# Channel attention folded into a two-MLP kernel: half of the fold moved between the first quad's products, the first tokens loaded during the gram, and up weights prepared quad by quad

## The reference

```python
# q, k, v: (1, 6016, 256); both MLPs: 256 -> 2048 -> 256
qn = q / (np.linalg.norm(q, axis=1, keepdims=True) + 1e-06)
kn = k / (np.linalg.norm(k, axis=1, keepdims=True) + 1e-06)
s = kn.transpose(0, 2, 1) @ qn / tau          # 256 x 256
a = np.exp(s - s.max(-1, keepdims=True)); a /= a.sum(-1, keepdims=True) + 1e-09
x = (v @ a).reshape(6016, 256)
x = np.square(np.maximum(x @ moe_w_in, 0.0)) @ moe_w_out
h = x @ moe2_w_in
y = np.maximum(0.01 * h, h) @ moe2_w_out
```

## Time and profile before

| | |
|---|---|
| median of 3 runs | 1052.86 us (1052.44 to 1053.63) |
| the profiled execution's own time | 1053.86 us |
| its span, first to last instruction | 1052.1 us |
| PE / DVE / ACT busy | 1026.6 / 735.7 / 673.0 us (98% / 70% / 64%) |
| mean granted TensorE clock | 0.995 |
| DMA | 69.24 MB, mean 66 GB/s |

### The profile page before, as it was taken

The page is one execution under the profiler, slowest core; times in us unless marked ns, Lnnn a source line. Parts: engine busy times, 40 slices in busy tenths (PEclk is TensorE's granted clock), DMA queues, the critical chain, the costliest instruction groups (busy, mean ns, idle before and its releaser), DMA issues.

```text
span 1052.1 us, 13051 instructions
## 1 busy us (share of the span) xinstructions
PE 1026.6 (98%) x4590; PEld 862.5 (82%) x4590; DVE 735.7 (70%) x1168; ACT 673.0 (64%) x1156; POOL 0.8 (0%) x7
## 2 busy tenths in 40 slices
PE   7978999999999999999999999999999999999998
PEld 6856788888888888888888888888888888888886
DVE  6887766766766666666656767767767767767665
ACT  6667767777777777777766555555555555555553
POOL 0000000000000000000000000000000000000000
PEclk9998999999999999999999999999999999999999
DMA  8730011203103113014436002002002001000001
GB/s 294 256 117 22 30 48 42 75 25 129 62 35 133 45 51 134 31 65 149 165 114 205 1 1 79 1 1 74 5 1 70 9 1 66 14 0 20 20 1 41
DMA packets 32400, 69.24 MB, mean 66 GB/s; under 512 B 2640, under 2 KB 16976, under 8 KB 32336
## 3 DMA queue, kind: packets, MB, share of 16 engines
q1 hardware_dynamic: 32336, 68.43, 19.2%
HBM read 44.56 MB, written 23.86 MB: 65 GB/s over the span
## 4 chain that ended last, share of the span: by engine, by line
PE 94%; DVE 2%; DMA 2%; ACT 1%; issue 1%; SPq 0%; ACTq 0%; DVEq 0%
PE bank L421 30%; PE bank L423 30%; PE bank L422 30%; PE bank L428 3%; DMA raw<-in_vT 1%; DMA qk<-in_k 1%; DVE xop_lo L846 0%; ACT win_hi L610 0%; DVE win_lo L872 0%; DVE g L990 0%; DVE wi_lo L777 0%; DVE wout_lo L877 0%; ACT wi_hi L576 0%; DVE folded L913 0%; ACT L580 0%
## 5 line engine op out<-in xcount | busy, mean ns | idle before, releaser
L672 ACT ACTIVATE g_hi<-g 128x496 fp32r<-128x496 f32 (+1 forms) x384 | 237.3, 618 | 208.5 <-DVE g L947 76.5
L937 DVE TENSOR_TENSOR g_lo<-g,g_hi 128x496 fp32r<-128x496 f32 (+1 forms) x384 | 260.1, 678 | 145.7 <-ACT g_hi L672 144.9
L421 PE MATMUL bank<-g_hi,wout_hi 128*128 128x496 f32 (+1 forms) x768 | 296.5, 386 | 0.0
L422 PE MATMUL bank<-g_lo,wout_hi 128*128 128x496 f32 (+1 forms) x768 | 296.3, 386 | 0.0
L423 PE MATMUL bank<-g_hi,wout_lo 128*128 128x496 f32 (+1 forms) x768 | 296.2, 386 | 0.0
L421 PE MATMUL bank<-xop_hi,win_hi 128*128 128x496 f32 (+1 forms) x672 | 260.8, 388 | 11.5 <-DVE g L990 9.0
L422 PE MATMUL bank<-xop_lo,win_hi 128*128 128x496 f32 (+1 forms) x672 | 259.9, 387 | 0.0
L423 PE MATMUL bank<-xop_hi,win_lo 128*128 128x496 f32 (+1 forms) x672 | 259.9, 387 | 0.0
L422 PEld LDWEIGHTS bank<-g_lo,wout_hi 128*128 128x128 f32 x768 | 144.5, 188 | 27.0
L423 PEld LDWEIGHTS bank<-g_hi,wout_lo 128*128 128x128 f32 x768 | 144.4, 188 | 27.1
L421 PEld LDWEIGHTS bank<-g_hi,wout_hi 128*128 128x128 f32 x768 | 144.5, 188 | 27.0
(11 more groups left out here) (99 smaller groups left out, 670.7 us busy)
## 6 DMA issues: line engine op xcount, KB each, us to landing
up_parts<-park_up SPq DMA_DIRECT2D x8, 896.0 KB, 4.4
qk<-in_q SPq DMA_DIRECT2D x15, 384.0 KB, 3.7
qk<-in_k SPq DMA_DIRECT2D x15, 384.0 KB, 5.1
stage_o<-in_w_out SPq DMA_DIRECT2D x16, 256.0 KB, 3.8
down_parts<-park_down SPq DMA_DIRECT2D x8, 512.0 KB, 2.9
raw<-in_vT SPq DMA_DIRECT2D x8, 496.0 KB, 5.9
x_tiles<-out_buf SPq DMA_DIRECT2D x8, 496.0 KB, 2.8
raw<-x_tiles SPq DMA_DIRECT2D x8, 496.0 KB, 4.2
```

Of the source, the lines that this page charges most:

```text
L421: pe.matmul(out, a_hi, b_hi, start=start and i == 0, stop=False, **more)
L422: pe.matmul(out, a_hi, b_lo, start=False, stop=False, **more)
L672: act.activation(g_hi[:, tile, 0:W], g[:, tile, 0:W], ACT.Copy).then_inc(g_hi_made[tile], 1)
L937: dve.tensor_tensor(g_lo[:, tile, 0:W], g[:, tile, 0:W], g_hi[:, tile, 0:W].bitcast(F32), ALU.subtract).then_inc(g_split[tile], 1)
```

## The change

- The tokens of group 0 (`raw0`, two DMAs of 512 KB) are loaded during the gram, after the tenth chunk; those of group 1 as soon as the gram is ready. Both have places of their own in SBUF; w_in1 gets four stage buffers in place of three, and its four loads wait for nothing.
- The sums of squares (L455 before) are put on PE before the last gram chunk, and `q_row` before the last gram tile. DVE copies `q_row` to SBUF (`q_bc`) and makes the scaled gram in one instruction a block in place of two. Six matmuls whose result nobody reads (`KEEP_WARM`) stand between the gram and the transposes.
- PE runs only units 0 to 3 of the fold before window 0. Units 4 to 7 stand between window 0's products, each of which waits only for the token block and the weights that it reads.
- `folded` is laid out by quad, and `up_add`, `up_high`, `up_low` work on one quad: 128 and 384 elements in place of 256 and 512+256; quad 0 before window 0, quad 1 in it, and quad n+1 in window n. Of the scaling, DVE keeps one unit and ACT takes seven. The second MLP's quads go through the same functions.
- The blocks of tokens are split in another order (`SPLIT_ORDER`), that in which window 0 reads them. Group 1's sums are made from window 1 on.

```diff
-STAGES = 3
+KEEP_WARM = 6
 CHUNK = 1024
-EARLY_CHUNKS = 2
...
-SPLIT_ORDER = (B11, B21, B22, T1, T2, T4, T3)
+SPLIT_ORDER = (B11, T1, T2, B21, T3, B22, T4)
+SUM_ORDER = (T1, T2, T3, T4)
...
-            with sp.Fori(1, QK_ROUNDS) as r:
+            def load_raw0():
+                for j in range(2):
+                    sp.dma_start(raw0[:, 2 * j:2 * j + 2, 0:width(0)], vT_b[:, :, tokens(0, j)]).then_inc(raw_loaded, 16)
...
-                for slot in range(QK_SLOTS):
-                    c = r * QK_SLOTS + slot
-                    sp.wait_ge(chunk_used, c - QK_SLOTS + 1)
-                    sp.wait_ge(chunk_squared, c - QK_SLOTS + 1)
-                    load_chunk(c, slot)
+            for c in range(QK_SLOTS, QK_CHUNKS):
+                sp.wait_ge(chunk_used, c - QK_SLOTS + 1)
+                sp.wait_ge(chunk_squared, c - QK_SLOTS + 1)
+                load_chunk(c, c % QK_SLOTS)
+                if c == 2 * QK_SLOTS - 1:
+                    load_raw0()
...
-                if n >= STAGES:
-                    sp.wait_ge(w_split, n - STAGES + 1)
...
-            sp.wait_ge(gram_ready, 1)
-            load_raw(0)
             load_down(0)
             load_down(1)
+            sp.wait_ge(gram_ready, 1)
+            load_raw(1)
             load_up(0)
...
+                if slot == QK_SLOTS - 1:
+                    pe.wait_ge(constants, 2)
+                    pe.wait_ge(chunk_added, QK_CHUNKS + 1 + QK_TILES)
+                    for i in range(2):
+                        for b in range(CB):
+                            last = pe.matmul(sums[:, i, b, :], sq_sum[:, i, 0, b * P:(b + 1) * P], ones[:, 0:2],
+                                             start=True, stop=True)
+                    last.then_inc(sums_ready, 1)
...
+            gram_tile(edge[:, 0, 1, :], edge[:, 1, 1, :], False, True).then_inc(gram_ready, 1)
+
+
+            pe.wait_ge(w_hi, 1)
+            for i in range(KEEP_WARM):
+                pe.matmul(fold[0], wi1_hi[:, 0, 0:P], wi1_hi[:, 0, 0:UNIT], start=True, stop=True)
...
+            def wait_weights(Q, split):
+                G, quad = divmod(Q, QUADS)
+                if G == 0:
+                    pe.wait_ge(up_split, 2 * quad + split)
+
...
+            def first_window():
+                W = width(0)
+                def x_ready(part):
+                    pe.wait_ge(x_split, SPLIT_ORDER.index(part) + 1)
+                wait_weights(0, 1)
+                x_ready(B11)
+                pe.wait_ge(fold_scaled[0], 1)
+                product(0, bank_a[:, 0:W], A11, B11, True).then_inc(p1_ready, 1)
+                fold_unit(4)
+                wait_weights(0, 2)
+                x_ready(T1)
+                pe.wait_ge(fold_scaled[1], 1)
+                product(0, bank_c[:, 0:W], S1, T1, True).then_inc(p5_ready, 1)
+                fold_unit(5)
+                x_ready(T2)
+                pe.wait_ge(seeded, 1)
+                product(0, bank_d[:, 0:W], S2, T2, False).then_inc(u2_ready, 1)
+                x_ready(B21)
+                product(0, bank_a[:, 0:W], A12, B21, False).then_inc(c11_ready, 1)
+                fold_unit(6)
+                x_ready(T3)
+                pe.wait_ge(u2_kept, 1)
+                product(0, bank_d[:, 0:W], S3, T3, False).then_inc(u3_ready, 1)
+                x_ready(B22)
+                pe.wait_ge(p5_kept, 1)
+                product(0, bank_c[:, 0:W], S4, B22, False).then_inc(p35_ready, 1)
+                fold_unit(7)
+                x_ready(T4)
+                pe.wait_ge(c22_made, 1)
+                product(0, bank_d[:, 0:W], A22, T4, False).then_inc(c21_ready, 1)
+
+
             def window(Q):
                 G, quad = divmod(Q, QUADS)
                 W = width(G)
...
+            for u in range(UNITS // 2):
+                fold_unit(u)
...
+            x_high(0, 0)
+            weights_hi(0)
+            weights_hi(1)
+            act.wait_ge(sums_ready, 1)
+            act.activation(norm[:, :, :], sums[:, :, :, 0], ACT.Sqrt).then_inc(rooted, 1)
+            act.activation(warm[:, 1:2], ones[:, 0:1], ACT.Exp)
+            x_high(0, 1)
+            weights_hi(2)
+            weights_hi(3)
...
+                act.wait_ge(e_inv_ready, 1)
+                x_high(0, 2)
+                x_high(0, 3)
+                fold_scale(0, 0)
+                up_high(0)
+                fold_scale(1, 0)
+                up_sums_high(0)
+                act.wait_ge(p1_ready, 1)
+                act.wait_ge(fold_scaled[0], 2)
+                act.activation(bank_d[:, 0:W], bank_a[:, 0:W], ACT.Copy).then_inc(seeded, 1)
+                fold_scale(1, 1)
+                x_high(0, 4)
+                x_high(0, 5)
+                act.wait_ge(p5_ready, 1)
+                act.activation(p5[:, 0:W], bank_c[:, 0:W], ACT.Copy).then_inc(p5_kept, 1)
+                act.wait_ge(u2_ready, 1)
+                act.activation(u2[:, 0:W], bank_d[:, 0:W], ACT.Copy).then_inc(u2_kept, 1)
+                x_high(0, 6)
+                up_high(1)
+                act.wait_ge(c11_ready, 1)
+                square(0, C11, bank_a, c11_relu)
+                fold_scale(2, 0)
+                fold_scale(2, 1)
+                g_high(0, C11)
+                down_high(0)
+                up_sums_high(1)
+                g_high(0, C22)
+                fold_scale(3, 0)
+                act.wait_ge(c21_ready, 1)
...
+            def up_add(n):
+                a11, a12, a22, a21 = (up_blocks(n)[:, i, :] for i in range(4))
+                s1, s2, s3, s4 = (wsum[:, n % 2, i, :] for i in range(4))
+                if n < QUADS:
+                    dve.wait_ge(fold_scaled[0], n // 2 + 1)
+                    dve.wait_ge(fold_scaled[1], n // 2 + 1)
+                else:
+                    dve.wait_ge(up_loaded, 32 * (n - QUADS + 1))
+                dve.tensor_tensor(s1, a21, a22, ALU.add).then_inc(up_sums, 1)
+                dve.tensor_tensor(s3, a11, a21, ALU.subtract).then_inc(up_sums, 1)
+                dve.wait_ge(up_sums, 4 * n + 1)
+                dve.tensor_tensor(s2, s1, a11, ALU.subtract).then_inc(up_sums, 1)
+                dve.wait_ge(up_sums, 4 * n + 3)
...
+            weights_lo(1)
+            dve.wait_ge(q_row_ready, 1)
+            dve.tensor_copy(q_bc[:, :], q_row).then_inc(q_bc_ready, 1)
...
+                dve.scalar_tensor_tensor(out=s_neg[:, i, :], in0=gram[i], scalar=inv[:, 1, i:i + 1], in1=q_bc[:, :],
+                                         op0=ALU.mult, op1=ALU.mult).then_inc(link, 1)
...
+            weights_lo(2)
+            fold_scale_first()
+            up_low(0)
+            up_add(0)
             x_low(0, 1)
-            dve.wait_ge(e_inv_ready, 1)
-            fold_scale(0)
-            up_add(0)
+            up_sums_low(0)
             x_low(0, 2)
+            weights_lo(3)
+            x_low(0, 3)
+            x_sum(0, T3)
+            x_low(0, 4)
+            x_low(0, 5)
             x_sum(0, T4)
...
+                if G == 0 and 0 < quad < QUADS - 1:
+                    up_sums_low(quad + 1)
...
+                if G == 0 and 0 < quad < QUADS - 1:
+                    up_add(quad + 1)
+                    up_low(quad + 1)
```

445 lines of the change are left out of this document (200 added, 245 removed).

## The result

The changed kernel takes 1045.51 us (median of 4 runs, 1044.72 to 1047.55) where the kernel before takes 1053.11 beside it: a ratio of 0.9931, interval 0.9914 to 0.9948. Timed again later it took 1045.7 (1044.13 to 1046.65), ratio 0.9937 (0.9919 to 0.9955). So it is faster, by 7.6 us and not by the 13.2 forecast, and 1039.7 and the whole range to 1042.9 are too low. Profile against profile it is 1053.86 - 1044.72 = 9.1 us.

The account below looks back on a forecast made before the run. PE, busy 98%, was taken to bound the kernel, with 16.8 us of surplus from fold to window 8. Waits 8.0, clock 3.4, restarts 1.4 and start 0.45 gave 13.2 off 1052.86: 1039.7 us, range 1038.6 to 1042.9.

Parts of the forecast that it names:

- From window 8 on: Window 8 to the end: PE's list and work unchanged and without waits, so nothing added or given back.
- End of the gram: Last gram chunks to fold: token load delays chunk 12 by 0.8 us, squares ready at 47.1, fold at 55.1, 0.45 earlier.
- Cost nothing: Between gram and transposes: six idle matmuls (1.4 us) end at 53.6, before the transposes can start, so cost no time.
- Fold and window 0: Fold to window 0's end: first product at 60.7 without wait, then waits of 0.3 (u2) and 0.4 us (C22).
- Window 1: Window 1: PE waits 0.4 us before the first product and 2.3 us before the second, for quad 1's weights.
- Windows 2 to 7: Windows 2 to 7: DVE has 1.0 us to spare in each, so no PE wait; window 8 starts at 146.3.
- Rival 2: Before window 1's second product or ahead of the sums: clock falls again, costing 1.4 to 2.0, up to 3.0 us; chance 0.24.
- Profile to median: Whole kernel: the median lies 1.0 us below the profiled time, as before, so 1052.86 - 13.2 = 1039.7 us.
- rival 1: End of the gram: token load holds up the chunks, fold at 56.95, 1.85 us more, 1041.6 us; chance 0.17.
- Rival 3: Later windows: weights by the quad still late, the 3.5 us of waits in windows 3 and 5 stay, 1043.2; chance 0.07.
- Rival 4: Windows 2 to 7: DVE's list per window outgrows PE's, slower than before, 1053 us or more; chance 0.02.
- Rival 5: Gram and window 0 to 1 passage: no delay by the load, no last 0.4 us waits, 1038.8 us; chance 0.05.

Follow-up runs that it names:

- experiment 1: Changed kernel with DVE doing the next group's token sum and low part before the parked weights in groups 1 to 4: 1040.61 us, ratio 0.9892.
- before_q0a: Kernel before, with each group's first token conversion and sum behind the tiles PE waits for, from group 1, first MLP only: 1049.61 us, ratio 0.9973.
- experiment 6: Five end-of-gram variants, four on the changed kernel: token load moved (1044.15, 1045.29 us), sums after the last chunk (1043.87; 1035.51 on a later version), no idle matmuls (1044.55).
- before_sum_late: Kernel before with only group 1's token sums one window later in DVE's order, windows 1 to 4 instead of 0 to 3: 1051.26 us, ratio 0.9984.

## Why the prediction was wrong, by its own steps

It fell short by 1045.5 - 1039.7 = 5.8 us: 4.0 in the profiled execution (1044.7 against 1040.7) and 1.8 in how I carried it to the median.

- **The step that failed**, and the largest of the misses: "From window 8 on PE's list and work are the same, and PE had no wait there, so nothing is added or given back". PE's list is the same, but the list of the engine it waits for is not. In DVE's `extras` the parked weights moved ahead of the token parts. The forecast compared what the two lists contain, not their order. This gave back 2.8 us: four waits with their restarts (window 10: 0.67 over 9.90), and a slow pace in the windows of group 1 behind them, less the one window of 10.33 that the kernel before had. Undoing the order takes off 4.9 us in the medians (experiment 1).
- *Windows of 10.05 us.* The kernel before already ran windows 16 to 39 at the slow pace (the first of them 10.33), and the forecast didn't see that: it read 399.87 of 400 us busy, and a slower pace doesn't show as idle time. 3.9 us lay there (before_q0a gains 3.3 in the medians).
- *End of the gram*: fold forecast at 55.1, found at 56.24 and at 55.47 when taken again, so this step is off by 0.4 to 1.1. From sums to fold I had 8.0 and it is 8.1. Off was the squares' time: 47.1 against 48.1 and 47.35. In the first profile chunk 12's high part starts at 38.00 where it was 36.27, 1.7 late and not 0.8. Much of that is chance: the forecast's own delay of 0.8 us is what the profiles show on the mean (experiment 6), but it was added to the earliest of the five profiles without the load, whose squares are ready at 46.31, where the five go up to 47.32. The gain of 0.45 is not there: the fold starts at 55.11 to 55.69 in the four profiles of the kernel before and its versions, and at 54.86 to 56.54 in the ten at full clock with early sums. "Cost nothing" for the idle matmuls is right, and no worth of theirs is shown either.
- *Fold and window 0*: right. First product at 61.81 with no wait, 5.57 us behind the fold (5.6 forecast). The wait for u2 (0.3) is there, though too short for the list of waits: its matmul starts at 69.08, 0.51 behind the one before, where 0.23 is free. The one for C22 is 0.4 as forecast.
- *Window 1*: right. 0.17 before the first product (0.4), 2.17 before the second (2.3).
- *Windows 2 to 7*: right, no wait. Window 8 starts at 147.53 (146.3): all of the 1.2 is the fold's, 91.3 us from fold to window 8 where 91.2 was forecast.
- *Rival 2, the clock*: not in the profiled execution, but real. Its two places are those where it was found in other executions, and its price, 1.4 to 2.0, up to 3.0, was found as 1.3 to 2.9 us. The row that spoke against it, a wait of 2.41 us with no half clock behind it, was one draw too: before_sum_late and before_q0a have the same wait (2.5 and 2.6 us), and the clock is 0.50 from 73 to 75 us in both. (The forecast's first stretch at half clock, 55.0 to 58.7, is in truth 55.4 to 58.8, which changes nothing in its sum.) The Trainium skill, TensorE: Matmul & The Clock Gate, Part 1: The HAM clock gate, says that the moment may differ from run to run; that the clock fell in 4 of 10 profiles with the same wait agrees.
- *Profile to median*: "1.0 lower, and I carry that over". The changed kernel's profile is its lowest run, 0.8 under the median, the kernel before's lies 0.8 to 1.0 above. Executions differ by the pace and by the clock, and one profile shows one draw. That is 1.8 us.
- *Rivals 1, 3, 4 and 5*: rival 1 had the sums at 48.9 and the fold at 56.95; the truth lies between it and the forecast. (By its own 3 us of delay the squares would be ready at 49.3, not 48.9.) Rival 3 said later waits stay for weights of windows 3 and 5; later waits came, elsewhere and from another cause. Rival 4 had the right engine, DVE, and the wrong windows. Rival 5, better than forecast, did not come.

The better version is best_q0b: token parts ahead of parked weights, window 0 and 1 reordered, the first token sum of a first-MLP group later, column sums after the last chunk. 1035.51 us, ratio to the kernel before 0.9845 (0.9825 to 0.9865), 10 us under the changed kernel timed beside it.

## What to carry to other kernels

Where a change rewrites an engine's list, compare the order of that list in every stage that runs it, also far from the place the change is about: an item that waits for another engine must not stand ahead of work that is ready and that a third engine needs. A stage "busy 100%" can still run at two paces; take the length of equal windows from their starts, not from the idle time. And before carrying a gain from one profile to a median, look at how far the runs of the kernel spread and why.
